# Windowed attention into two expert layers: q unmasked, keys in one tile, one fused op for bias and minimum, short rows of weight DMAs

## The reference, cut to what matters

```python
# attention, q, k, v: (2, 8, 768, 64); 32-token blocks, window 16
k_sum = k.reshape(B, H, nb, block, D).max(axis=3)        # 24 block keys
v_sum = v.reshape(B, H, nb, block, D).mean(axis=3)       # 24 block values
scores_l = where(|i - j| < window, scale * q @ k.T, -1e9)
scores_s = scale * q @ k_sum.T + log(block)
a = softmax(concat([scores_l, scores_s], -1))
x = (a @ concat([v, v_sum])).reshape(1536, 512)
# experts: 8 of 512 -> 1024 -> 512, one expert for each token
do = x @ w_skip > 0;  logits = x @ w_gate;  e = argmax(logits)
x[do] += softmax(logits)[e] * (relu(x[do] @ w1[e]) @ w2[e])
# dense layer, 512 -> 2048 -> 512
h = x @ w_in;  out = (h * cos(h)) @ w_out
```

## Time and profile before

| | us |
|---|---|
| median of 3 runs | 577.41 (577.04 to 580.43) |
| profiled execution | 577.29 |
| its span | 575.5 |
| PE busy | 506.0 (88%) |
| DVE busy | 280.8 (49%) |
| ACT busy | 231.4 (40%) |
| POOL busy | 131.1 (23%) |

### The profile page before, as it was taken

How to read it: one execution, slowest core, us unless ns; L and a number is a source line. 1 busy time by engine, 2 the same in 40 slices (tenths; PEclk the granted TensorE clock), 3 DMA queues, 4 the chain that set the end, 5 groups by cost and what they waited for, 6 DMA issues and landing times.

```text
span 575.5 us, 11095 instructions
## 1 busy us (share of the span) xinstructions
PE 506.0 (88%) x4357; PEld 414.1 (72%) x4357; DVE 280.8 (49%) x520; ACT 231.4 (40%) x555; POOL 131.1 (23%) x174
## 2 busy tenths in 40 slices
PE   5797999974925999695978898999999999999996
PEld 5787899964713666463856667888888888888885
DVE  3553455533000000054047888767767676676664
ACT  2454565530202333231135445444444445444442
POOL 3568567413321222122231331000000000000000
PEclk9798899975985999998869999999999999999999
DMA  6566577999999170877240000000500000200001
GB/s 208 134 210 210 194 224 219 274 342 394 395 370 397 70 305 16 325 285 302 65 168 1 1 0 1 0 1 23 197 1 1 0 1 0 75 1 1 0 1 73
DMA packets 39598, 78.93 MB, mean 137 GB/s; under 512 B 4544, under 2 KB 18880, under 8 KB 39552
## 3 DMA queue, kind: packets, MB, share of 16 engines
q1 hardware_dynamic: 37792, 73.30, 37.1%
q0 software_dynamic: 1760, 4.98, 2.4%
HBM read 65.95 MB, written 10.75 MB: 133 GB/s over the span
## 4 chain that ended last, share of the span: by engine, by line
PE 39%; DVE 7%; ACT 3%; issue 2%; DMA 1%; POOL 0%; POOLq 0%; DVEq 0%; ACTq 0%
PE bank L1063 13%; PE bank L1065 13%; PE bank L1064 13%; DVE turns L904 2%; DVE reduced L908 1%; DVE reduced L911 1%; ACT turns L657 1%; PE bank L1154 1%; DVE reduced L914 1%; DMA y_tokens<-y_out,row_of_slot_now 1%; DMA y_stage<-y_tokens 0%; DVE gT_lo L923 0%; ACT turns L664 0%; ACT wout_hi L638 0%; ACT h_copy L660 0%
## 5 line engine op out<-in xcount | busy, mean ns | idle before, releaser
L1063 PE MATMUL bank<-wout_hi,gT_hi 128*128 128x512 f32 x192 | 75.8, 395 | 6.9 <-DVE gT_lo L923 6.9
L1063 PE MATMUL bank<-x2T,win_hi 128*128 128x512 f32 x192 | 76.8, 400 | 1.4 <-DVE x2T L891 1.4
L1065 PE MATMUL bank<-x2T,win_lo 128*128 128x512 f32 x192 | 75.8, 395 | 0.0
L1064 PE MATMUL bank<-x2T,win_hi 128*128 128x512 f32 x192 | 75.7, 394 | 0.0
L1065 PE MATMUL bank<-wout_hi,gT_lo 128*128 128x512 f32 x192 | 74.8, 390 | 0.0
L1064 PE MATMUL bank<-wout_lo,gT_hi 128*128 128x512 f32 x192 | 74.8, 389 | 0.0
L664 ACT ACTIVATE turns<-reduced,half_pi 128x512 f32<-128x512 f32 x48 | 34.8, 725 | 82.7 <-DVE reduced L914 82.7
L904 DVE TENSOR_SCALAR turns<-turns 128x512 f32<-128x512 f32 x48 | 31.3, 652 | 60.6 <-ACT turns L657 60.6
L865 DVE CAST win_hi<-w_slot 128x1024 fp32r<-128x1024 f32 x8 | 5.4, 687 | 113.4 <-DMA w_slot<-weights 113.4
L657 ACT ACTIVATE turns<-bank,quarter 128x512 f32<-128x512 f32 x48 | 33.0, 687 | 62.1 <-PE bank L1065 62.1
L1063 PEld LDWEIGHTS bank<-wout_hi,gT_hi 128*128 128x128 f32 x192 | 36.0, 188 | 18.1 <-DVE gT_lo L923 10.7
(11 more groups left out here) (156 smaller groups left out, 870.2 us busy)
## 6 DMA issues: line engine op xcount, KB each, us to landing
w_slot<-weights SPq DMA_DIRECT2D x80, 512.0 KB, 15.8
q_raw<-q_T SPq DMA_DIRECT2D x8, 384.0 KB, 6.1
k_padded<-k_T SPq DMA_DIRECT2D x8, 384.0 KB, 5.3
v_tok<-v_pairs SPq DMA_DIRECT2D x8, 384.0 KB, 7.1
v_window<-v_pairs SPq DMA_DIRECT2D x8, 384.0 KB, 4.7
y_tokens<-zeros SPq DMA_DIRECT2D x6, 512.0 KB, 9.9
x_tile<-x_plain SPq DMA_DIRECT2D x12, 256.0 KB, 5.3
y_stage<-y_tokens SPq DMA_DIRECT2D x12, 256.0 KB, 4.0
```

The lines of the kernel that those rows point to most:

```text
L1063: te.matmul(out_ap, a[0], b[0], start=start, stop=False)
L1064: te.matmul(out_ap, a[0], b[1], start=False, stop=False)
L1065: return te.matmul(out_ap, a[1], b[0], start=False, stop=stop)
```

## The change

q is no longer masked by POOL: DMAs write each head's half of the rows of `qbd`, whose other half DVE has zeroed once. Block keys and windows of a tile lie in one tile `keys` of 128 columns, which POOL fills by two copies (`make_keys`, two steps ahead); the first pair's are made by DVE. Scores of the two heads are products of their own, into the two halves of PSUM's partitions. Scale stands in the bias (`nbias` is divided by it), and bias and minimum are one `tensor_tensor_reduce` for each tile. x transposed and its logits come from one product with the identity and the gate weights side by side (`identw`); DVE adds the logits to a tile in SBUF (`add_logits`). v is summed by DVE over 8 tokens (`sum_tokens`) in front of one product. q is loaded one pair ahead. Weight chunks wait for the chunk two before them (`chunk_wait`), and no longer for `blocks_ready`; 12 chunks instead of 16 go beside attention, four behind it. `y_free` starts at four. POOL holds one gather more in flight, and the first four loads of y are issued by ACT instead of SP.

```diff
--- before.py
+++ after.py
...
-BESIDE = 2
+BESIDE = (1, 2, 2, 2, 2, 1, 1, 1)
+VTOK = 8
...
+        def chunk_wait(eng, s, load, c):
+
+            eng.wait_ge(w_loaded[s][c % 2], 16 * (NCH // 2 * load + c // 2 + 1))
+
         def weights_wait(eng, e, half):

-            eng.wait_ge(w_loaded[SLOT_OF[e]][half], 64 * (1 + e // SLOTS))
+            for c in (NCH // 2 * half + 2, NCH // 2 * half + 3):
+                chunk_wait(eng, SLOT_OF[e], e // SLOTS, c)
...
             def load_q(i):
-                ge(sp, q0_placed, min(i - 1, 1))
-                ge(sp, q_placed, GPP * (i - 2))
-                sp.dma_start(qraw[i % 2][:, :], qT[i, :, :]).then_inc(q_loaded[i % 2], 16)
+                ge(sp, scores_ready, GPP * (i - 1))
+                for head in range(2):
+                    h = slice(D * head, D * (head + 1))
+                    sp.dma_start(qbd[i % 2][h, head, :], qT[i, h, :]).then_inc(q_loaded[i % 2], 16)
...
-            def load_chunk(src, s, c):
-                sp.dma_start(wslot[s][:, c, :], weights[NCH * src + c, :, :]).then_inc(w_loaded[s][c // 4], 16)
+            def load_chunk(src, s, c, load=0):
+
+
+                if c >= 2:
+                    chunk_wait(sp, s, load, c - 2)
+                sp.dma_start(wslot[s][:, c, :], weights[NCH * src + c, :, :]).then_inc(w_loaded[s][c % 2], 16)
...
+            load_k(1)
             sp.wait_ge(pads_ready, 1)
             load_windows(0)
-            load_k(1)
             load_q(1)
             load_vtok(1)
             place_vsum(0)
...
+                if i > 0 and i + 1 < PAIRS:
+                    load_q(i + 1)
                 if i + 2 < PAIRS:
-                    load_q(i + 2)
...
-                for n in range(BESIDE * i, BESIDE * (i + 1)):
+                for n in range(sent, sent + BESIDE[i]):
                     load_chunk(n // NCH, n // NCH, n % NCH)
+                sent += BESIDE[i]
...
+            for n in range(sent, 2 * NCH):
+                load_chunk(n // NCH, n // NCH, n % NCH)
             sp.wait_ge(xps_ready, STEPS)
-            for c in range(NCH):
-                load_chunk(2, SLOT_OF[2], c)
-            for k in range(NCH):
-                sp.wait_ge(blocks_ready, k + 1)
-                if k == NCH // 2:
+            for e in (2, 3, 4):
+                if e == 4:
                     sp.wait_ge(x_stored, 16 * XSTORES)
                     sp.wait_ge(zero_stored, 16 * (NT // 2))
-                for c in (2 * k, 2 * k + 1):
-                    load_chunk(3 + c // NCH, SLOT_OF[3 + c // NCH], c % NCH)
+                for c in range(NCH):
+                    load_chunk(e, SLOT_OF[e], c)
...
-            for done, src, s in ((1, 5, 0), (2, 6, 1), (3, 7, 3), (4, E, 4), (6, E + 1, 0)):
+            for done, src, s, load in ((1, 5, 0, 1), (2, 6, 1, 1), (3, 7, 3, 1), (4, E, 4, 1), (6, E + 1, 0, 2)):
                 sp.wait_ge(expert_done, done)
                 for c in range(NCH):
-                    load_chunk(src, s, c)
-            sp.wait_ge(y_all, 1)
-            for q in range(TPG):
-                load_y(q, q)
+                    load_chunk(src, s, c, load)
...
+            pool.sem_inc(y_free, CG)
...
-            def place_q(s):
+            def make_keys(s):
+

                 i, gr = s // GPP, s % GPP
-                pool.wait_ge(q_loaded[i % 2], 16 * (i // 2) + 16)
+                pool.wait_ge(ksum_ready, i + 1)
                 ge(pool, scores_ready, s - 2 * GPP + 1)
-                src = qraw[i % 2][:, GT * QT * gr:GT * QT * (gr + 1)].rearrange("p (t q) -> p t q", q=QT)
-                dst = qbd[i % 2][:, GT * gr:GT * (gr + 1), :]
-                g.tensor_scalar(dst[:, :, 0:QT], src, head_mask[:, 0:1], None, ALU.mult)
-                g.tensor_scalar(dst[:, :, QT:2 * QT], src, head_mask[:, 1:2], None, ALU.mult).then_inc(q_placed, 1)
+                own = kpad[i % 3][:, GT * QT * gr:GT * QT * (gr + 1)]
+                windows = bass.AP(own.tensor, own.offset, [own.ap[0], [QT, GT], [1, WIN]])
+                dst = keys[i % 2][:, GT * gr:GT * (gr + 1), :]
+                g.tensor_copy(dst[:, :, NSUM:COLS], windows)
+                g.tensor_copy(dst[:, :, 0:NB], ksum[i % 2][:, :].rearrange("p (o n) -> p o n", o=1)
+                              .broadcast_to([P, GT, NB])).then_inc(keys_made, 1)
...
             for s in range(STEPS):
                 normalise(s, s % 2, s % 3)
-                if s + GPP < STEPS:
-                    place_q(s + GPP)
+                if GPP <= s + 2 < STEPS:
+                    make_keys(s + 2)
...
-            for k in range(NBLK + 2):
...
-                if k >= 2:
-                    pool.wait_ge(gathered[(k - 2) % 4], 16 * ((k - 2) // 4 + 1))
+                if k >= 3:
+                    pool.wait_ge(gathered[(k - 3) % 4], 16 * ((k - 3) // 4 + 1))
                     pool.sem_inc(blocks_ready, 1)
...
-                    pool.sem_inc(y_free, 1)
+                    if not isinstance(k, int):
+                        pool.sem_inc(y_free, 1)
...
+            act.wait_ge(y_all, 1)
+            for q in range(TPG):
+                src = yd[CG * P * (q + NBLK):CG * P * (q + NBLK + 1), :].rearrange("(p g) f -> p (g f)", g=CG)
+                act.dma_start(yst[q][:, :], src).then_inc(yst_loaded[q], 16)
...
+            def sum_tokens(i):
+
+                dve.wait_ge(vtok_loaded[i % 2], 16 * (i // 2) + 16)
+                ge(dve, vs_ready, i - 1)
+                v.tensor_reduce(out=vred[i % 2][:, :], in_=vtok[i % 2][:, :, :].rearrange("p t d -> p d t"),
+                                axis=AX.X, op=ALU.add).then_inc(vred_ready, 1)
...
-                v.scalar_tensor_tensor(out=nsc[par][:, :, :], in0=sc_ps[par][:, :].rearrange("p (t c) -> p t c", t=GT),
-                                       scalar=-SCALE, in1=nbias[:, gr:gr + GT, :],
-                                       op0=ALU.mult, op1=ALU.add).then_inc(scores_read, 1)
-                dve.wait_ge(scores_read, s + 1)
-                v.tensor_reduce(out=nmin[:, par, :], in_=nsc[par][:, :, :], axis=AX.X, op=ALU.min)\
-                    .then_inc(nmin_ready, 1)
+                for t in range(GT):
+                    last = v.tensor_tensor_reduce(nsc[par][:, t, :], sc_ps[par][:, COLS * t:COLS * (t + 1)],
+                                                  nbias[:, gr + t, :], -SCALE, 3.0e38, ALU.add, ALU.min,
+                                                  nmin[:, par, t:t + 1])
+                last.then_inc(nmin_ready, 1)
...
+            def add_logits(s):
+
+                i, t = s // GPP, TPB * (s // GPP // PPB) + 2 * (s % GPP)
+                if s == STEPS - 1:
+                    dve.wait_ge(xtps_ready, STEPS)
+                else:
+                    dve.wait_ge(xt_copied, s + 1)
+                part = xt_ps[s % 2][:, 0:2 * (P + E + 1)].rearrange("p (t f) -> p t f", t=2)[:, :, P:P + E + 1]
+                if i % PPB == 0:
+                    v.tensor_copy(lg[:, t:t + 2, :], part).then_inc(lg_added, 1)
+                else:
+                    dve.wait_ge(lg_added, s)
+                    v.tensor_tensor(lg[:, t:t + 2, :], lg[:, t:t + 2, :], part, ALU.add).then_inc(lg_added, 1)
...
             for s in range(2):
-                v.memset(ksum[s][:, NB:NSUM], 0.0).then_inc(keys_padded, 1)
+                v.memset(keys[s][:, :, NB:NSUM], 0.0).then_inc(keys_padded, 1)
+            dve.wait_ge(keys_padded, 5)
+            make_summary(0)
+            own = kpad[0][:, 0:S]
+            v.tensor_copy(keys[0][:, :, NSUM:COLS], bass.AP(own.tensor, own.offset, [own.ap[0], [QT, TPP], [1, WIN]]))
+            dve.wait_ge(ksum_ready, 1)
+            v.tensor_copy(keys[0][:, :, 0:NB], ksum[0][:, :].rearrange("p (o n) -> p o n", o=1)
+                          .broadcast_to([P, TPP, NB])).then_inc(keys0_made, 1)
+            sum_tokens(0)
...
-                if s % GPP == 1 and s // GPP + 1 < PAIRS:
+                if s >= 6:
+                    add_logits(s - 6)
+                if s % GPP == 0 and s // GPP + 1 < PAIRS:
                     make_summary(s // GPP + 1)
+                if s % GPP == 2 and s // GPP + 1 < PAIRS:
+                    sum_tokens(s // GPP + 1)
...
+                if s < 2:
+                    pe.wait_ge(q_zeroed, s + 1)
                 if i == 0:
-                    pe.wait_ge(q0_placed, 1)
-                ge(pe, q_placed, s - GPP + 1)
+                    pe.wait_ge(keys0_made, 1)
                 if gr == 0:
-                    pe.wait_ge(ksum_ready, i + 1)
-                ge(pe, scores_read, s - 1)
+                    pe.wait_ge(q_loaded[i % 2], 32 * (i // 2) + 32)
+                ge(pe, keys_made, s - GPP + 1)
+                ge(pe, nmin_ready, s - 1)
                 for t in range(GT):
-                    q, n = qbd[i % 2][:, GT * gr + t, :], GT * gr + t
-                    te.matmul(sc_ps[par][:, COLS * t:COLS * t + NSUM], q, ksum[i % 2][:, :], start=True, stop=True)
```

(28 more changed lines are left out.)

122 lines of the change are left out of this document (61 added, 61 removed).

## The result

The kernel after takes 597.27 us (median of 4; before in the same comparison 577.9, 577.4 ahead of the prediction), a ratio of 1.0294, 95% interval 1.0209 to 1.0378. The prediction said 567 us, at most 585, and faster; the change makes the kernel slower.

The account below looks back on a forecast made before the run. PE was taken to bound attention, with DVE and POOL having slack, and the experts to lose 37 us to stops. Terms: 577.3 + 20 (attention) - 31 (experts) - 0.5 (gathers) + 1 (tail) = 566.8, said as 567; range 552 to 585.

Parts of the forecast that it names:

- The fused row: Attention, DVE: four fused bias-and-minimum ops take 1.4 us a step (0.9 to 1.8) against 1.33 before, so fusion gains nothing.
- The loop: Attention: POOL's keys for s+2 wait on scores of s+1, so steps run in series at 5.0 us each.
- The wait for q: Attention: q, loaded one pair ahead behind the value sum and chunks, lands late and adds 1.7 us a pair.
- the forecast case: Whole kernel: slower attention, much faster experts, 558 to 575 us; chance 0.42.
- the constants: Attention: POOL's 6 us of writing constants only partly fits the loop's waits, adding 2 us.
- the store: Attention, before the last pair: the 1.5 MB store of x lies in front of q, adding 2.5 us.
- The floor of 87 us: Experts: 18 tiles without a stop take 87 us in place of 124.35.
- I keep 6 us: Experts: idles at changes of expert and slow products behind them still cost 6 us, about half of before.
- idles stay: Rival, experts: PE loses all it loses now except the wait for y_free; gain 18 us, kernel 580; chance 0.12.
- The point from which weights bind: Experts: weights forecast at 1.6 us a chunk arrive in time, and bind only above 1.85 us a chunk.
- My rival: Weights bind: 2.4 us a chunk makes the sixth to eighth experts wait some 15 us, kernel 582; chance 0.08.
- the written sign of being wrong: Prediction is wrong if attention stays near 104 us or the experts stay above 105 us.

Follow-up runs that it names:

- e1: The kernel after, with q for pair i+2 loaded ahead of the value sum and the weight chunks: 567.05 us, 0.9814 of the kernel before.
- e10: The kernel after, with a pair's weight chunks issued behind the next pair's k, q and v, q still behind the value sum: 582.03 us, 1.0078.
- e11: e5 without loading weights of experts 5 to 7 and of the last product, so its output differs: 526.07 us, measured once.
- e4: The kernel after, with four weight chunks in flight in place of two: 583.21 us, 1.0106 of the kernel before.
- e7: The kernel after with q first, keys three steps ahead and no limit on weight chunks in flight: 538.24 us, 0.9328 of the kernel before.
- e5: The kernel after with q ahead of the chunks, keys three steps ahead and four weight chunks in flight: 537.01 us, 0.9314 of the kernel before.
- e6: The kernel before, with only y_free raised by four at POOL's start: 564.11 us, 0.977 of the kernel before.

## Why the prediction was wrong, step by step

Against the profiled 591.3 us the forecast of 566.8 is 24.5 us short: 2.0 up to the first expert product (+21.5 measured, +20 and -0.5 forecast), 18.4 in the experts (-12.6, forecast -31), 4.8 in the tail (+5.8, forecast +1), -0.7 in the last layer. So the step that failed is the experts, and the tail with late weights as the cause in part; attention's sum came out close, in part by luck, since its terms were not.

**Scores, fused ops, keys.** Scores 1.14 us (forecast 1.2), keys 0.77 (0.8), inverse and normalise as forecast. The fused row was put at 1.4 and takes 0.85, under its lower bound of 0.9: the four overlap to 0.21 us apart though one lasts 0.29, and the reads of the accumulator fit in. The Trainium skill ("VectorE: DVE Perf Modes", section "Two Vector instructions with no wait between them") has such an op as two instructions; the trace agrees, with 96 reads of 0.08 us, but the fused ops start 0.21 us apart with the reads beside them, where I let the reads lift the value. "The fusion gains nothing" was wrong by 0.48 us a step.

**The loop** is there: PE waits for POOL's keys, and a step takes 4.2 us in place of 5.0: 0.55 us from the fused row, the rest from keys with the hop behind them (0.77, forecast 0.9), normalise and scores.

**The wait for q** was sized at 1.7 us a pair and costs 5.4. Three things make the difference: with a loop of 4.2 the scores could start 7.3 us (2 x 4.2 - 1.14) behind the read of step 3i+1, not 8.8 (60.36 + 7.3 = 67.6, q lands at 71.76): +1.5; q lands 9.56 us behind the value sum, not 8.4 as before, and the value sum 1.84 behind that read, not 2.1: +0.9; and the wait drops the clock, as the earlier trace rows showed for 2.99 us: the scores then take 0.9 us more and the next step 0.4. I had written that a slower loop hides the wait and named both as steadier together, and did not carry the slowed clock of a pair's restart into the forecast case, although the row for it was there. A pair of 18.0 in the mean (16.5, 18.1, 17.6, 18.2, 18.5 and 19.2) against 16.5 gives 9 us in six pairs. The forecast had 4.5 of them in terms of their own, 2 for the constants and 2.5 for the store: the constants vanish in the wait for q, and of the store at most the last pair's 19.2 us is seen. With a fourth score 2.6 us later (21.6, forecast 19) and the last two steps 1.6 us shorter, the last step's first fused op is 5.5 us later than forecast (138.04, forecast 132.5). From there to the first expert product it is 3.1 us less than before, where +0.5 was forecast, which gave most of that back; no run shows why. e1 and e10 show this cause: q early takes 26.8 us off attention.

**The experts.** The floor of 87 us was right: e11 measures 87.4. What failed is "I keep 6 us" for idles and slow products, from the assumption that a short row of chunks shortens the fetches. The kernel after has 12.3 us of issue idles, 4.3 of waiting for weights, 1.0 for xT_tile, and 94.74 us of busy PE against 88.03 at full clock in e11, 6.7 for slow products: 87.4 + 12.3 + 4.3 + 1.0 + 6.7 = 111.7 of 111.8. So the 6 us kept were 24. The idles were 14.2 us before. With the waits for weights they are 16.6 us here, 13.1 with four chunks in flight (e4) and 15.9 without a limit (e7), so a shorter row gained nothing; without weights in the later experts they are 7.4 (e11). The low end of my own bounds, -18, was the case of "idles stay" at 0.12; even that was 5.4 us too much. It counted "only the wait for y_free" as 18 us, where PE waits 15.3 in the trace of before, and late weights take 4.3 back. The Trainium skill ("Runtime: NRT & Kernel Launch", section "Instruction fetch mechanics") has a taken branch to code outside the fetched pages wait for a DMA. The trace agrees in that e5 has seven idles of 0.3 to 4.2 us, most of them near a change of expert, and waits there for nothing that the profile shows; that weights in flight lengthen them only e11 shows, and that they are such fetches no run shows.

**The weights.** 1.6 us a chunk was forecast, with 0.65 for each of 14 gathers beside; 2.39 was measured with the gathers in it, so (66.94 - 9.1) / 28 = 2.07 without them. The point from which weights bind was given as 1.85; by the forecast's own numbers (99 us for 52 chunks and 9.1 us of gathers) it is 1.73, and 2.07 is above both. The row I scaled, a 256 KB store in 2.1 us, ran with nothing beside it; a chunk of 512 KB lands in 4.7 us here, in place of my 2.75. The rule in the Trainium skill that I cited ("DMA: Bandwidth & Descriptors", section "Anatomy of one DMA") gives 3.2 us, an estimate, and the page fits it to DMAs that GpSimd issues, where SP issues these; the measurement decides. My rival had this case at 2.4 us a chunk, 0.08 and 15 us: e4 gains 14. But the rival looked for all of it in the sixth to eighth experts; the experts give 6.8, with a wait of 4.3 us, and the tail 7.3, where I had put +1 for weights in flight beside the loads of y. The mechanism was in the text, its chance was far too low.

**What was right:** the gap of 15 us behind y_free goes (11.8 us in the experts, e6); no other y_out wait comes; PE's clock in attention is under 0.92; and the change is decided by attention against experts. Attention near 126 us and experts above 105 us: the second was the written sign of being wrong.

What stays open: why PE's idles in the experts are still 7.4 us in sum without weights in the later half, why routing is 3 us shorter, and how attention's other parts (scores in halves, one product for x and logits) share the 23.7 us that attention gains once q and keys are early; no run separates them.

## What to carry to other kernels

When a load moves from two pairs ahead to one, write down its whole queue, from the wait that releases it to its landing, against the shortest step that the rest allows, and charge the clock of the restart with each wait. Two bounds in one loop hide each other: an edit that gave 5.4 us alone, not clear of noise, gave 16.5 once the first was gone. And a limit on transfers in flight must be priced by their landing in company (4.7 us for 512 KB here), not by a transfer that ran alone.

## What the runs showed of the hardware

- Sixteen DMA engines can be busy 1.00 of the time at very different rates: 251 GB/s in e5's attention, where 12,838 of 17,151 packets are under 2 KB, and 362 GB/s in its early experts (127.7 to 182).
- Fused two-input ops with a minimum over 128 columns last 0.29 us, start 0.21 us apart, and have their accumulator reads of 0.08 us beside them.
- A PE idle of 5.4 us in attention was followed by 6.6 us at a granted clock of 0.56 (71.7 to 78.3 in the kernel after), and attention had 0.84; with the waits for q gone (e1) it had 0.93.
